# Moving the experts' hidden transposes from TensorE to a DMA round trip and VectorE

## The reference

```python
# n_tokens, d_model, experts, d_ff = 2304, 512, 8, 1024
noisy_logits = x @ w_gate + log1p(exp(x @ w_noise)) * noise
top2 = argpartition(-noisy_logits, 2, axis=1)[:, :2]
top2_w = softmax of the two chosen logits
for e in range(E):
    for k in range(2):
        mask = top2[:, k] == e
        h = np.maximum(x[mask] @ w1[e], 0.0)
        out[mask] += top2_w[mask, k, None] * (h @ w2[e])
```

## Time and profile before

| what | value |
|---|---|
| time, median of 3 runs | 1078.3 us (1078.17 to 1080.13) |
| the profiled execution's own time | 1076.49 us |
| its span, first to last instruction | 1074.7 us |
| TensorE (PE) busy | 1062.6 us, 99% |
| VectorE (DVE) busy | 588.3 us, 55% |
| ScalarE (ACT) busy | 327.8 us, 31% |
| GpSimd (POOL) busy | 386.8 us, 36% |

### The profile page before, as it was taken

One profiled execution on the slowest core, in us unless ns is written; L12 is line 12 of the kernel. 1 busy time (PEld: TensorE's weight loads), 2 busy tenths in 40 slices (PEclk: granted clock), 3 DMA queues, 4 the chain that ended last, 5 costly groups with the idle time before them and its releaser, 6 DMA issues.

```text
span 1074.7 us, 20097 instructions
## 1 busy us (share of the span) xinstructions
PE 1062.6 (99%) x6053; PEld 931.9 (87%) x6054; DVE 588.3 (55%) x1226; ACT 327.8 (31%) x724; POOL 386.8 (36%) x358
## 2 busy tenths in 40 slices
PE   8999999999999999999999999999999999999998
PEld 7878999999999999999988888888888888888886
DVE  6887434363363463453447775565555556555554
ACT  7987122342342432432352111020302021110222
POOL 4667990030030030120185415070706143250486
PEclk9999999999999999999999999999999999999999
DMA  7985525411311311211074536172616344331676
GB/s 218 276 264 190 176 89 187 127 59 30 118 59 30 117 59 30 98 59 30 26 250 153 161 80 174 39 207 46 195 47 161 85 117 127 82 104 39 168 242 235
DMA packets 199634, 133.18 MB, mean 124 GB/s; under 512 B 128752, under 2 KB 161408, under 8 KB 199584
## 3 DMA queue, kind: packets, MB, share of 16 engines
q1 hardware_dynamic: 177728, 75.14, 25.9%
q10 hardware_dynamic: 16032, 38.47, 10.9%
q0 software_dynamic: 5824, 18.95, 5.1%
HBM read 85.87 MB, written 42.73 MB: 120 GB/s over the span
## 4 chain that ended last, share of the span: by engine, by line
PE 93%; POOL 2%; DMA 2%; issue 1%; DVE 1%; SPq 0%; POOLq 0%; ACT 0%; DVEq 0%
PE bank L873 28%; PE bank L1041 20%; PE bank L1062 20%; PE bank L905 14%; PE bank L1075 3%; PE bank L817 2%; PE bank L844 2%; PE bank L827 1%; POOL token_rows_a L750 1%; PE bank L811 1%; DMA token_rows_b<-expert_rows,slots_u 1%; PE bank L958 1%; DMA q_sb<-in_qT 1%; POOL token_rows_a L763 1%; DMA k_sb<-in_kT 0%
## 5 line engine op out<-in xcount | busy, mean ns | idle before, releaser
L873 PE MATMUL bank<-x_parts,mlp_weights 128*128 128x384 f32 x1704 | 309.4, 336 | 0.0
L873 PEld LDWEIGHTS bank<-x_parts,mlp_weights 128*128 128x128 f32 x1704 | 298.3, 188 | 5.3
L1041 PE MATMUL bank<-expert_parts,xT_high 128*128 (+1 forms) x688 | 216.6, 396 | 0.0
L1062 PE MATMUL bank<-expert_parts,hT_high 128*128 (+1 forms) x688 | 212.2, 390 | 0.0
L732 POOL TENSOR_TENSOR expert_parts<-raw_expert_a,expert_parts 128x512 fp32r<-128x512 f32 x64 | 81.4, 1305 | 234.3 <-ACT expert_parts L1372 232.0
L905 PE MATMUL bank<-mlp_weights,hidden_parts 128*128 128x512 f32 x648 | 162.1, 395 | 0.0
L1062 PEld LDWEIGHTS bank<-expert_parts,hT_high 128*128 128x128 f32 x688 | 129.0, 188 | 26.9 <-issue 0.4
L1041 PEld LDWEIGHTS bank<-expert_parts,xT_high 128*128 128x128 f32 x688 | 125.8, 188 | 24.3 <-issue 0.4
L905 PEld LDWEIGHTS bank<-mlp_weights,hidden_parts 128*128 128x128 f32 x648 | 120.2, 188 | 23.4 <-issue 1.0
L1041 PE MATMUL bank<-expert_parts,xT_low 128*128 (+1 forms) x344 | 134.4, 391 | 0.0
L1062 PE MATMUL bank<-expert_parts,hT_low 128*128 (+1 forms) x344 | 134.2, 390 | 0.0
(11 more groups left out here) (220 smaller groups left out, 1230.1 us busy)
## 6 DMA issues: line engine op xcount, KB each, us to landing
raw_expert_a<-in_w ACTq DMA_DIRECT2D x32, 512.0 KB, 4.6
raw_expert_b<-in_w ACTq DMA_DIRECT2D x32, 512.0 KB, 4.2
x_row<-routed_rows SPq DMA_DIRECT2D x172, 64.0 KB, 2.6
expert_rows<-y_row SPq DMA_DIRECT2D x43, 256.0 KB, 2.0
expert_rows<-zeros SPq DMA_DIRECT2D x4, 2304.0 KB, 11.9
v_sb<-in_v SPq DMA_DIRECT2D x32, 256.0 KB, 3.9
q_sb<-in_qT SPq DMA_DIRECT2D x15, 288.0 KB, 3.7
k_sb<-in_kT SPq DMA_DIRECT2D x15, 288.0 KB, 4.1
```

Of the source, the lines that this page charges most:

```text
L873: last = nc.tensor.matmul(bank[:, 0:CHUNK], w_sb[:, i, wp, at:at + P], xp[:, par, part, k, :], start=n == 0, stop=n == 3 * KB - 1)
L1041: last = nc.tensor.matmul(ps[half][:, 0:512], (xTh, xTl)[xp][:, buf, k, :], ew_sb[:, bass.ds(slot, 1), wp, k * F2 + half * 512:k * F2 + ha ...
L1062: last = nc.tensor.matmul(y_bank(t)[:, 0:D], (hTh, hTl)[hp][:, f, :], ew_sb[:, bass.ds(slot, 1), 2 + wp, f * D:(f + 1) * D].rearrange("p a ...
```

## The change

For tiles 4 to 41 TensorE no longer transposes. VectorE writes the ReLU's result with its columns in another order: the 32-column blocks of equal place q in their 128 columns stand together. SP moves each half of `relu` (128 x 512) to DRAM (`hidden_by_blocks`, two copies by the parity of t), waits for that, and brings it back with four transfers, one for each quarter of the partitions, into the SBUF tile `hidden_blocks` (`move_hidden`). VectorE then transposes 32 x 32 blocks from there into bank 2 or 3 (`dve_turn`), where TensorE wrote before. Tiles 0 to 3 and 42 keep TensorE's transposes.

VectorE's order in a tile becomes first half of `dve_hT` of t-1, first half of `dve_relu` of t, second half of each. `relu` may be overwritten when its half has gone out (`hidden_out`). In SP's queue a tile is now: both halves of t out, each behind its ReLU; both halves of t in; the rows of t+3; the store of t-1. SP's and TensorE's loops are written out for all tiles. TensorE reads the table's entries for t+1 between the two halves of down of t-1.

```diff
@@ sync
-            with sp.Fori(0, (ETILES - 5) // 2) as m:
-                for a in range(2):
-                    load_rows(2 * m + (5 + a), (5 + a) % 2)
-                    store_rows(2 * m + (2 + a))
+            def move_hidden(t):
+                for half in range(2):
+                    sp.wait_ge(relu_done, 2 * t + half + 1)
+                    sp.dma_start(hs_dram[t % 2, :, half * 512:half * 512 + 512], relu[:, half * 512:half * 512 + 512]
+                                 ).then_inc(hidden_out[half], 16)
+                for half in range(2):
+                    sp.wait_ge(hidden_out[half], 16 * (t + 1 - FIRST_TURNED))
+                    sp.wait_ge(hT_done, 2 * t - 1 + half)
+                    blocks = hs_dram[t % 2, :, half * 512:half * 512 + 512].rearrange("(s r) (q n) -> q r s n", s=BLOCKS, q=BLOCKS)
+                    for q in range(BLOCKS):
+                        sp.dma_start(hB[q * BLOCK:(q + 1) * BLOCK, half * 512:half * 512 + 512].rearrange(
+                            "r (s n) -> r s n", s=BLOCKS), blocks[q]).then_inc(hidden_in[half], 16)
+            for t in range(FIRST_TURNED, ETILES - 3):
+                move_hidden(t)
+                load_rows(t + 3, (t + 3) % 2)
+                store_rows(t - 1)
@@ tensor
-                now = entries(t)
-                before = entries(t - 1)
-                pe_hT(pe, t - 1)
-                pe_up2(pe, t, buf, *now)
-                pe_down2(pe, t - 1, *before)
+            for t in range(5, ETILES - 1):
+                pe_up2(pe, t, t % 2, *now)
+                pe_down2(pe, t - 1, *before, (0,))
+                later = entries(t + 1)
+                pe_down2(pe, t - 1, *before, (1,))
+                before, now = now, later
@@ vector
+        def dve_turn(dve, t, half):
+            dve.wait_ge(hidden_in[half], 16 * BLOCKS * (t + 1 - FIRST_TURNED))
+            dve.wait_ge(hTl_done, 2 * t - 1 + half)
+            nc.vector.transpose(ps[2 + half][:].rearrange("p (f s c) -> p f s c", s=BLOCKS, c=BLOCK),
+                                hB[:, half * 512:half * 512 + 512].rearrange("p (s f c) -> p f s c", s=BLOCKS, c=BLOCK)
+                                ).then_inc(hT_done, 1)
@@ dve_relu
+                if not isinstance(t, int) or t > FIRST_TURNED:
+                    dve.wait_ge(hidden_out[half], 16 * (t - FIRST_TURNED))
+                to, bank = relu[:, half * 512:half * 512 + 512], ps[half][:]
+                if not isinstance(t, int) or FIRST_TURNED <= t < ETILES - 1:
+                    to = to.rearrange("p (q f c) -> p q f c", q=BLOCKS, c=BLOCK)
+                    bank = bank.rearrange("p (f q c) -> p q f c", q=BLOCKS, c=BLOCK)
@@ vector's tile
-                dve_hT(dve, t - 1)
-                dve_relu(dve, t)
+                dve_hT(dve, t - 1, (0,))
+                dve_relu(dve, t, (0,))
+                dve_hT(dve, t - 1, (1,))
+                dve_relu(dve, t, (1,))
                 dve_xT(dve, t + 1, buf, earlier)
                 dve_y(dve, t - 1)
```

More of the change, by code:

```diff
@@ L57, in attention_moe_kernel @@
     ye_dram = nc.dram_tensor("expert_rows", [ETILES * P, D], F32).ap()
+    hs_dram = nc.dram_tensor("hidden_by_blocks", [2, P, F2], F32).ap()
     ROW = 512
@@ L92, in attention_moe_kernel @@
     y_sb = at("y_sb", [P, CHUNK_TILES, D], F32, STAGE_OFF + 2 * 4096)
+    hB = at("hidden_blocks", [P, F2], F32, STAGE_OFF + 2 * 4096)
+    assert F2 <= CHUNK_TILES * D
     yT_sb = at("yT_sb", [P, CHUNK_TILES, KB, P], F32, STAGE_OFF + D * 4)
@@ L350, in attention_moe_kernel @@
         half_done = sem("half_done")
+        hidden_out = [sem(f"hidden_out_{i}") for i in range(2)]
+        hidden_in = [sem(f"hidden_in_{i}") for i in range(2)]
         y_row_done = sem("y_row_done")
@@ L402, in parts @@
             return EARLY_LOWS * min(i + 1, EARLY_BLOCKS) + LOWS * max(i + 1 - EARLY_BLOCKS, 0)
+        FIRST_TURNED = 4
         TO_T, TO_PV = 3, 4
@@ L590, in _ @@
             store_rows(1)
-            with sp.Fori(0, (ETILES - 5) // 2) as m:
-                for a in range(2):
-                    load_rows(2 * m + (5 + a), (5 + a) % 2)
-                    store_rows(2 * m + (2 + a))
-            for t in range(ETILES - 3, ETILES):
-                store_rows(t)
+            load_rows(5, 1)
+            store_rows(2)
+            load_rows(6, 0)
+            def move_hidden(t):
[14 more added lines that the diff above has]
+                store_rows(t - 1)
+            for t in range(ETILES - 3, ETILES - 1):
+                move_hidden(t)
+                store_rows(t - 1)
+            store_rows(ETILES - 2)
+            store_rows(ETILES - 1)
             sp.wait_ge(y_row_out, 16 * ONE + 16 * ETILES)
@@ L1109, in entries @@
                 return entry(pe, t + T_SLOT, 1), entry(pe, t + T_E, E - 1)
-            def tile(t, buf):
-                now = entries(t)
-                before = entries(t - 1)
-                pe_hT(pe, t - 1)
-                pe_up2(pe, t, buf, *now)
-                pe_down2(pe, t - 1, *before)
-                return now
             fourth = entries(3)
             pe_up2(pe, 3, 1, *fourth)
-            fifth = entries(4)
-            pe_up2(pe, 4, 0, *fifth, (0,))
+            before = entries(4)
+            pe_up2(pe, 4, 0, *before, (0,))
             pe_hT(pe, 3)
[L1124 to L1129, removed]
+            pe_up2(pe, 4, 0, *before, (1,))
+            pe_down2(pe, 3, *fourth, (0,))
+            now = entries(5)
+            pe_down2(pe, 3, *fourth, (1,))
+            for t in range(5, ETILES - 1):
[4 more added lines that the diff above has]
+                before, now = now, later
             t = ETILES - 1
-            now = entries(t)
-            pe_hT(pe, t - 1)
             pe_up2(pe, t, t % 2, *now)
@@ L1811, in dve_xT @@
             nc.vector.tensor_tensor(xTl[:, buf], x_T, xTh[:, buf].bitcast(F32), ALU.subtract).then_inc(xTl_done, 1)
+        def dve_turn(dve, t, half):
[4 more added lines that the diff above has]
+                                ).then_inc(hT_done, 1)
         def dve_hT(dve, t, halves=(0, 1)):
             for b in halves:
+                if not isinstance(t, int) or FIRST_TURNED <= t < ETILES - 1:
+                    dve_turn(dve, t, b)
                 dve.wait_ge(hT_done, 2 * t + b + 1)
@@ L1830, in dve_relu @@
                 dve.wait_ge(up_done, 2 * t + half + 1)
-                if not (isinstance(t, int) and t == 0):
+                if isinstance(t, int) and 0 < t <= FIRST_TURNED:
                     dve.wait_ge(hT_done, 2 * t - 1 + half)
-                nc.vector.tensor_scalar(relu[:, half * 512:half * 512 + 512], ps[half][:], 0.0, None, ALU.max
-                                        ).then_inc(relu_done, 1)
+                if not isinstance(t, int) or t > FIRST_TURNED:
+                    dve.wait_ge(hidden_out[half], 16 * (t - FIRST_TURNED))
+                to, bank = relu[:, half * 512:half * 512 + 512], ps[half][:]
+                if not isinstance(t, int) or FIRST_TURNED <= t < ETILES - 1:
+                    to = to.rearrange("p (q f c) -> p q f c", q=BLOCKS, c=BLOCK)
+                    bank = bank.rearrange("p (f q c) -> p q f c", q=BLOCKS, c=BLOCK)
+                nc.vector.tensor_scalar(to, bank, 0.0, None, ALU.max).then_inc(relu_done, 1)
         def dve_y(dve, t):
@@ L1871, in dve_experts @@
             for t, extra in ((4, dve_places), (5, dve_combine)):
-                dve_hT(dve, t - 1)
-                dve_relu(dve, t)
+                if t == FIRST_TURNED:
+                    dve_relu(dve, t, (0,))
+                    dve_hT(dve, t - 1)
+                else:
+                    dve_hT(dve, t - 1, (0,))
+                    dve_relu(dve, t, (0,))
+                    dve_hT(dve, t - 1, (1,))
+                dve_relu(dve, t, (1,))
                 dve_xT(dve, t + 1, (t + 1) % 2, (t + 1) // 2)
```

## The result

The changed kernel takes 1101.3 us (median of 4 runs, 1098.4 to 1102.9) against 1079.2 for the one before on the same chip: a ratio of 1.020, 95% interval 1.0175 to 1.0227. It is slower by 22 us, where 14.5 us of gain were forecast, in a range of 1046 to 1084 us. The profiled execution took 1101.53 us with a span of 1099.7.

The account below looks back on a forecast made before the run. The prediction took TensorE, busy 99% of the span, to bound the kernel: 28.5 us gained less 14 of stalls beside weight loads gives -14.5 us, from 1078.3 to 1063.8, say 1064 us, range 1046 to 1084.

Parts of the forecast that it names:

- TensorE's gain: Experts' stage: 38 tiles without transposes save 33.1 us; less 3.5 at the tail and 1.1 at tiles 4 and 5, 28.5.
- tiles 4 and 5: Start of the turned tiles: VectorE still at dve_places, so 0.65 us gained out of 1.74, 1.1 lost.
- code and reads: TensorE's written-out tiles and register reads between halves of down: costed at nothing, reads at most 11 us in all.
- the cover: VectorE in each tile: 8.2 us of work in 10.9, results about 2.3 us before TensorE wants them, so added work hides.
- SP's issues: SP's queue: inward moves issued at a pitch of 0.55 us, with 0.43 and 0.79 kept as the ends.
- SP's own work a tile: SP's queue: outward 0.8, eight inward pitches, x_row 3.1 and store 0.4 sum to 8.7 us (7.7 to 10.6), below 10.9.
- the slower rival: SP's queue paces every tile: at a pitch of 1.0 us a tile takes 12.3, the kernel 1111 us; chance 0.20.
- The stalls beside weight loads: TensorE in five weight-load bursts: idle 2.8 us a burst, between 1.4 and 3.5, 14 us in all.
- the round: From one ReLU through DRAM to the next: 10.25 us in quiet stretches, 13.1 beside weight loads, 2.2 too much.
- The traffic sum of 316 GB/s: DMA in weight-load bursts: the moves' 96 GB/s added to 219, where no slice shows over 276, so landings must grow.
- The end: Tail from tile 38: GpSimd's gathers pace it; four tiles' transposes bring nothing, and a TensorE stall up to 3.5 us costs nothing.
- the rival of the saturated memory path: Memory path in weight-load bursts: 5 x 5.5 = 27 us of stalls, 1077 us, hardly a change; chance 0.14.

Follow-up runs that it names:

- e2_no_trip: The changed kernel without any move of the hidden blocks, VectorE turning them straight out of relu (output not the reference's): 1050.4 us, 0.972 of the kernel before.
- e3: The changed kernel with all moves made but unused, VectorE turning out of relu without waiting for a landing (output not the reference's): 1093.7 us, ratio 1.013 to before.
- e7: The changed kernel, but with tiles 36 to 41, those beside the gathers, transposed by TensorE as before: 1095.9 us, ratio 1.016 to the kernel before.
- e14: The changed kernel with an eighth of each weight piece loaded from the third expert on, and tiles 36 to 41 transposed by TensorE: 1062.8 us, 0.985 of before.

## Why the prediction was wrong

*TensorE's gain* was right. 28.5 us were forecast before stalls, and e2_no_trip measures 28.6 (1079.0 - 1050.4). Its parts hold in kind: tiles of 10.88 us, tiles 4 and 5 gaining 0.6 (69.0 to 68.4), nothing gained at the end, nothing from code and reads. That the sum agrees to 0.1 us is luck: the profiled spans differ by 25.7 (1074.7 - 1049.0), as the profiled execution before was 2.7 us under its median.

*VectorE* was right: the turn has a mean of 722 ns and the reordered ReLU 0.68 to 0.69, inside the cover.

*SP's issues* were right in size: a pitch of 0.46 for 0.55. The first step that failed is the sum built on them. "SP's own work a tile is then ... 4.3 + 8p = 8.7 us, below 10.9" adds issues and leaves out that SP stands in line for the first outward landing. The measured pitch makes it 8.0; the landing's 2.4 us take the place of the 0.8 put in for outward issues, 1.6 more, and register reads ahead of x_row add 0.7. The quiet round from 671.70 to 682.13 is 10.4 us, so a late turn regains 0.45 us a tile and not 0.65, and beside loads 705.30 to 718.33 is 13.0, over TensorE's 10.9. So SP's queue is a circle of its own beside loads, though not by the pitch that the slower rival named. e3 shows it: with the data's circle cut, tiles beside loads still take 14 to 15 us.

*The stalls beside weight loads* were right in place and kind and too small in size: 2.8 us a burst forecast, 40 us over some five and a half bursts measured, 7 us a burst. This is the second step that failed, and the largest term. Three things are in it: landings of 4.2 to 6.6 outward and 4.7 to 6.9 inward, where 4.2 and 4.1 were put into the round and 6 was only the upper end; SP's circle, which holds back the recovery; and the clock, which was not costed at all. By the two stretches above, TensorE waits 28 us of the 40, 5 a burst, which is the upper end of the prediction's own range; the other 12.5 are slower work, with the clock at its lower level behind the waits (3.2 us behind the one of 6.5). How the 28 divide between the landings and SP's circle was not separated. The traffic sum of 316 GB/s was right (below), and I should have let it decide the landings.

```profile
663.00:675.00 12.00, 12.00 (x54) 9.91 (x53) 9.40 (x15) 0.00 (x0) 0.00 (x0) 0.99 0.53 156
706.00:720.00 14.00, 11.29 (x48) 8.61 (x47) 8.21 (x13) 5.26 (x5) 14.00 (x13) 1.00 1.05 323
```

*The end* was wrong, and it is the third step: "a TensorE stall of up to that much there costs nothing either" allowed 3.5 us, but from y_row 36 to y_row 42 the changed kernel took 75.6 us, for 60.1 without the trip (65.2 before). The gathers keep the DMA engines busy there (a DMA share of 0.84 from y_row 36 to the end), and no slower landing was costed beside them. e7's end, 72.1 us, gives the 10 us back.

In mechanism the rival of the saturated memory path came nearest, with 27 us of stalls for the 28 that TensorE waits in the middle; its time, 1077, lacks the clock and the end. In time the slower one did, with 1111, by the wrong mechanism: the outward issues took 0.32 to 0.47 us, the inward ones 0.43 in the median, with one of 1.9 as the longest. What stays open is the 9.6 us of e14's middle, e7's longer middle, and the division named above.

The Trainium skill (DMA: Bandwidth & Descriptors, "Issuing engines are not separate DMA queues") says that transfers issued by different engines run on the same 16 DMA engines and interleave. The trace agrees: beside ACT's loads SP's outward landings go from 2.4 to as much as 6.6 us.

## What to carry to other kernels

Where work goes from the bounding engine to a DMA round trip, draw each circle that the trip closes, through the data (result, out, in, next result) and through the in-order queue that issues it with every landing it stands for, and compare each with the period in the busiest stretch of the DMA engines, not in the quiet one. Add the new traffic to the old before taking a landing from the trace. When a circle overruns only in part, send half of the work through it and leave the stretches with other traffic alone: here that turned 22 us of loss into 11 us of gain. And where the bounding engine is TensorE, put its clock into the price of a stall.

## What the hardware showed unexpectedly

Landings of 256 KB to DRAM rise from 2.4 to as much as 6.6 us while the DMA share is near 1 (1.05 at 323 GB/s). One wait of 6.5 us on TensorE costs 9.7, since its clock is at 0.50 for the next 6 us. The Trainium skill (TensorE: Matmul & The Clock Gate, "Part 1: The HAM clock gate") describes throttling as the default state that activity releases; this row agrees. Spreading the same weight loads over nearly twice the time left the middle as it was (368.5 us both).
